# One link fewer before the flag, the spread of two integers as a 128-column product, a mask of GpSimd behind VectorE's, and one copy moved to VectorE

## The chip, the cores and the metric

The kernel runs on one core of a Trainium2 chip. The metric is the device time of one execution, in microseconds (us); lower is better. Engines are called TensorE (PE, with its weight loads as PEld), VectorE (DVE), ScalarE (ACT), GpSimd (POOL) and SyncE (SP, which here only issues transfers).

## What is computed

Attention followed by two feed-forward blocks, all in float32:

```python
scores = q @ k^T / sqrt(64)                   # 2 batches, 8 heads, 768 rows, head size 64
rel = i - j
keep = (j < n_global) | ((rel >= 0) & (rel < n_local))
dist = where(j < n_global and not local, n_local, |rel|)
scores = where(keep, scores - 2**-(h + 1) * dist, -1e9)     # h = 0..7, one slope per head
x = softmax(scores) @ v                       # reshaped to 1536 x 512
x = silu(x @ w_in1) @ w_out1                  # 512 -> 2048 -> 512
y = (h * clip(h + 3, 0, 6) / 6) @ w_out2, with h = x @ w_in2
```

n_global is 8 and n_local is 96, but they are int64 inputs that the kernel reads when it runs.

## The kernel before, in words

**Attention.** The 16 heads are 8 pairs; each pair has 6 tiles of 128 query rows. A unit u is one query tile of one pair of heads (48 units). Since only a band and a few global columns survive the mask, a unit computes 128 x 256 scores per head (128 x 128 in the first tile of a pair). This "banded" path holds if n_global is at most 32 and n_local is from 1 to 97; otherwise a "general" path runs. The choice is made on the device: VectorE computes a flag from the two integers, and every engine waits for it (`flag_ok`), loads it into a register and branches (`either`, L229 to L236).

**The start.** SyncE fetches the integers (L242). VectorE turns them into float32 (L531), writes three derived numbers in the same one-partition row (L532 to L534, each raising `row_ok`), and computes the flag in a chain of three dependent operations (L535, L536, L537), each waiting for the one before. TensorE multiplies idle tiles of ones meanwhile (L1058, four before and two behind), and between them the spread product (L1062): ones times a 128 x 5 tile `rows` whose first partition holds the five numbers, which puts them on all partitions. VectorE copies them from PSUM to `nums` (L544).

**The masks.** m_base holds, for each of 384 columns, minus eight times the distance or a very large negative number. VectorE makes its last 128 columns, OWN (L562, L564, L567, and L568 on 32 columns, which raises `own_ok`), and multiplies them by the slope of head 0 (L571). GpSimd makes the first 256, BAND (L427 on 32 columns, L430 on 256, and L433 on 32, which raises `band_ok`), with a clipped distance from ScalarE (L912). Then it multiplies them by the slope of head 1 (L436, `bias_band1`), and waits for own_ok before it makes the biases of the further heads (L330). VectorE multiplies BAND by the slope of head 0 (L575) after band_ok. ScalarE multiplies OWN by the slope of head 1 (L915) after own_ok.

**The flow of a unit.** TensorE's scores (L1088 for units 0 and 1, L1076 for two units at a time); VectorE's negation (L623), which adds the bias and takes the maximum, per head; ScalarE's exponential (L842), per head; TensorE's transposes of the probabilities (L1100) into one of two PSUM banks; a copy of these into probsT by ScalarE (L853) or VectorE (L636); TensorE's product with v (L1124). GpSimd prepares and spreads the inverse sums (L316, L324), TensorE turns them (L1109), ScalarE copies them (L858), and VectorE scales the outputs (L641). Transposes of unit u wait for the copy of unit u-2, and values wait for the copies of their own units. The helper `copied(u)` (L225) gives the semaphore and value of unit u's copy. VectorE copies the odd units from 3 on, ScalarE the even ones and unit 1.

**What sets the order.** Every engine's instructions are written out by hand, in `banded()` of each engine, and run strictly in that order; semaphores hold them back. The negation of unit u may start when the exponentials of unit u-3 are done, and scores of units 2r and 2r+1 when the negations of units 2r-2 and 2r-1 are.

**Feed-forward.** 32 steps, each of seven products of quarter matrices (L1152) and the product with w_out (L1234, L1243), on float32 split into a high and a low part. TensorE runs them back to back; VectorE, ScalarE and GpSimd split weights and apply the activation. The outputs are collected in y_out, which nothing uses before the second block, apart from the ones of the idle products (in y_out[:, 0, 0:128]).

Of the kernel before, what the change touches and what calls it, by code (L numbers as in the profile page):

```python
# [9 lines left out]
ALU = mybir.AluOpType  # L10
ACT = mybir.ActivationFunctionType

P = 128
# [11 lines left out]
GLOB = 32  # L25
KS = P + GLOB
KW = NT * KS - GLOB
MAXLOC = 97
MASKED = -1.0e9
NEVER = -1.0e30  # L30
# [41 lines left out]
def build(nc, qT, kT, v, w_in1, w_out1, w_in2, w_out2, counts, out):  # L72
    outer = ExitStack()
    with outer:
        def sb(name, shape, dt=F32, ctx=outer):
            return ctx.enter_context(nc.sbuf_tensor(name, shape, dt))
# [14 lines left out]
        wo_raw = sb("wo_raw", [P, 2, 2 * DM])  # L91
        ident = sb("ident", [P, P])
        words = sb("words", [1, 4], I32)
        rows = sb("rows", [P, 9])
        cnt = rows[0:1, :]
        nums = sb("nums", [P, 5])
        flag = sb("flag", [1, 1], I32)
        slope = sb("slope", [P, 2 * NH])
# [45 lines left out]
        g_hi = sb("g_hi", [P, 2, 2, 2 * TB], F32R)  # L144
        g_lo = sb("g_lo", [P, 2, 2, 2 * TB], F32R)
        y_out = sb("y_out", [P, NT, DM])

        ps = outer.enter_context(nc.psum_tensor("ps", [P, 8, 512], F32))

# [74 lines left out]

        def copied(u):  # L225

            return (pt_dve, u // 2) if u % 2 and u > 1 else (pt_act, u + 1 if u < 2 else u // 2 + 2)

        def either(eng, banded, general):  # L229

# [73 lines left out]
        def _(pool):  # L304
# [117 lines left out]
            def banded():  # L422

                key, far, glb = m_tmp[1], m_tmp[3], m_tmp[4]
                pool.wait_ge(nums_ok, 1)
                pool.wait_ge(iota_ok, MW_IOTAS)
                nc.gpsimd.tensor_scalar(glb[:, BAND_GLOB], key[:, BAND_GLOB], nums[:, 0:1], NEVER, ALU.is_ge,  # L427
                                        ALU.mult).then_inc(band_link, 1)
                pool.wait_ge(far_ok, 1)
                nc.gpsimd.tensor_tensor(m_base[:, BAND], rel8[:, BAND], far[:, BAND], ALU.subtract).then_inc(band_link, 1)  # L430

                pool.wait_ge(band_link, 2)
                nc.gpsimd.tensor_scalar(m_base[:, BAND_GLOB], glb[:, BAND_GLOB], nums[:, 3:4], 1.0, ALU.add,  # L433
                                        ALU.mult).then_inc(band_ok, 1)
                pool.wait_ge(band_ok, 1)
                nc.gpsimd.tensor_scalar(m_bias[:, 1, BAND], m_base[:, BAND], slope[:, 1:2], 1.0, ALU.mult,  # L436
                                        ALU.mult).then_inc(bias_band1, 1)
                pool.wait_ge(own_ok, 1)
                for r in range(NR):
                    if r < 3:  # L440
                        bias(2 * r + 2)
                        bias(2 * r + 3)
                    if r == 2:
                        spread(1)
                    elif r % 2 == 0 and r >= 4:
                        spread(r - 2)
                        spread(r - 1)
                    total(r)
                    if r == 1:
                        spread(0)  # L450
                    for kind, which, part in W_WORK.get(r, ()):
                        if kind == "s":
                            w_sum(which, part)
                        elif kind == "h":
                            w_high(which, part)
                        elif kind == "l":
                            w_low(which, part)
                        else:
                            wo_low(which)
                    for kind, which, half in X_WORK.get(r, ()):  # L460
                        if kind == "s":
                            x_sum(0, which, half)
                        elif kind == "h":
                            x_high(which)
                        else:
                            x_low(which)
                spread(NR - 2)
                spread(NR - 1)
                for n in (2, 3):
                    for half in range(2):  # L470
                        x_sum(0, n, half)
# [34 lines left out]
        def _(dve):  # L506
            links = [0]

            def link(ins):

                links[0] += 1
                ins.then_inc(chain, 1)
                dve.wait_ge(chain, links[0])

            nc.vector.memset(y_out[:, 0, 0:P], 1.0).then_inc(idle_ok, 1)
            nc.vector.memset(rows[:, 4:9], 0.0).then_inc(chain, 1)
            links[0] += 1
            for h in range(2 * NH):  # L520
                nc.vector.memset(slope[:, h:h + 1], 2.0 ** (-8.0 * (h % NH + 1) / NH)).then_inc(chain, 1)
# [7 lines left out]
            lowu = words[:, :].bitcast(U32).rearrange("p (n w) -> p n w", w=2)  # L529
            highi = words[:, :].rearrange("p (n w) -> p n w", w=2)  # L530
            link(nc.vector.scalar_tensor_tensor(cnt[:, 4:6], highi[:, :, 1], 4294967296.0, lowu[:, :, 0], ALU.mult, ALU.add))  # L531
            nc.vector.tensor_scalar(cnt[:, 6:7], cnt[:, 5:6], 0.0, None, ALU.max).then_inc(row_ok, 1)  # L532
            nc.vector.tensor_scalar(cnt[:, 7:8], cnt[:, 5:6], -8.0, 0.0, ALU.mult, ALU.min).then_inc(row_ok, 1)
            nc.vector.tensor_scalar(cnt[:, 8:9], cnt[:, 5:6], -0.5, -BEYOND, ALU.add, ALU.mult).then_inc(row_ok, 1)  # L534
            link(nc.vector.tensor_scalar(cnt[:, 0:1], cnt[:, 5:6], 1.0, None, ALU.is_ge))  # L535
            link(nc.vector.scalar_tensor_tensor(cnt[:, 0:1], cnt[:, 5:6], float(MAXLOC), cnt[:, 0:1], ALU.is_le, ALU.mult))  # L536
            nc.vector.scalar_tensor_tensor(flag[:, :], cnt[:, 4:5], float(GLOB), cnt[:, 0:1], ALU.is_le,  # L537
                                           ALU.mult).then_inc(flag_ok, 1)
            common = links[0]
            ng, nl = nums[:, 0:1], nums[:, 2:3]  # L540

            def numbers():
                dve.wait_ge(rows_ok, 1)
                nc.vector.tensor_copy(nums[:, :], ps[:, 1, 0:5]).then_inc(nums_ok, 1)  # L544
                dve.wait_ge(nums_ok, 1)

            def masks(link, rel, jj, loc, glb, keep, ngl, dist):
# [95 lines left out]
            def banded():  # L643
                numbers()
                base()

                def negations(r):
                    u = 2 * r
                    if u % NT == 0 and 0 < u < 4 * NT:
                        dve.wait_ge(bias_ok, 2 * (u // NT))  # L650
                    for k in (u, u + 1):
                        negated(k, 0)
                        negated(k, 1)

                negated(0, 0)
                dve.wait_ge(bias_own1, 1)
                negated(0, 1)
                band_bias()
                negated(1, 0)
                dve.wait_ge(bias_band1, 1)  # L660
                negated(1, 1)
                negations(1)
                inverse(0)
                negations(2)
                negations(3)
                inverse(1)
                copy_t(3)
                for m in range(2, NM):
                    negations(2 * m)
                    inverse(2 * m - 2)  # L670
                    if m == 2:
                        copy_t(4 * m - 3)
                    inverse(2 * m - 1)
                    negations(2 * m + 1)
                    if m > 2:
                        copy_t(4 * m - 3)
                    x_scaled(m - 2)
                    copy_t(4 * m - 1)
                inverse(NR - 2)
                inverse(NR - 1)  # L680
                x_low(0, T1)
                copy_t(NU - 3)
                x_scaled(NM - 2)
                x_low(0, B22)
                c_sum(0, 0, 1, p1_c, P2)
                copy_t(NU - 1)
                x_low(0, T3)
                x_low(0, T4)
                c_sum(0, 1, 0, p5_c, P7)
                silu(0, 0)  # L690
                c_sum(0, 2, 1, u2_c, P3)
                for n in range(1, 4):
                    silu(0, n)
                x_scaled(NM - 1)
# [131 lines left out]
        def _(act):  # L826
# [19 lines left out]
            def copy_t(u):  # L846
                act.wait_ge(pt_done, u + 1)
                at_least(act, pv_done, u // 2 - 2)
                src, dst = pt_bank(u), probsT[:, u % 6, :, :]
                if u % NT == 0:  # L850
                    src = src.rearrange("p (h a) k -> p h a k", h=2)[:, :, 1, :]
                    dst = dst.rearrange("p (h a) k -> p h a k", h=2)[:, :, 1, :]
                nc.scalar.activation(dst, src, ACT.Copy).then_inc(pt_act, 1)  # L853
# [55 lines left out]
            def banded():  # L909
# [10 lines left out]
                copy_t(1)  # L920
                exps(3)
                exps(4)
                copy_t(2)
                exps(5)
                exps(6)
                exps(7)
# [124 lines left out]
        def _(pe):  # L1051
# [3 lines left out]

            def busy(n):
                for _ in range(n):
                    nc.tensor.matmul(ps[:, 0, 0:P], y_out[:, 0, 0:P], y_out[:, 0, 0:P], start=True, stop=True)  # L1058

            busy(4)  # L1060
            pe.wait_ge(row_ok, 3)
            nc.tensor.matmul(ps[:, 1, 0:5], y_out[:, 0, 0:P], rows[:, 4:9], start=True, stop=True).then_inc(rows_ok, 1)  # L1062
            busy(2)
            pe.wait_ge(ident_ok, 2)

# [268 lines left out]
```

## Time and profile before

| | us |
|---|---|
| median of 3 runs | 587.07 (586.82 to 587.07) |
| the profiled execution's own time | 586.97 |
| its span, first to last instruction | 585.2 |
| TensorE busy in the span | 580.0 (99%) |
| VectorE busy | 361.9 (62%) |
| ScalarE busy | 335.5 (57%) |
| GpSimd busy | 266.7 (46%) |

The span is what the trace shows; the execution's own time has a little more around it. Busy time says how much of the span an engine had an instruction under way. It does not say what the others waited for: that is read from the chain of waits (followed back from the last instruction) and, where several engines work in turns, from the timeline. A fp32 product of TensorE appears as two records. The ends of TensorE's records are modelled, and its records overlap, as do those of VectorE and ScalarE by some hundredths where nothing is waited for.

### The profile page before, as it was taken

What the parts mean: (1) busy time and instruction counts of PE and PEld (TensorE: products, weight loads), DVE (VectorE), ACT (ScalarE), POOL (GpSimd) and SP (SyncE); (2) the same over time, 40 slices, a digit from 0 to 9 for tenths busy, and PEclk for the clock granted to TensorE, in tenths of its full rate; (3) what the DMA queues carried; (4) which work ended last, traced back from release to release, by engine and by line L of the source; (5) the groups of instructions that cost most, each with busy time, mean ns of one, the idle gap of its engine ahead of it and who ended that gap; (6) DMA issues with size and microseconds to landing.
All of it is one profiled execution on the core that took longest, in us unless ns stands there. A gap on an engine that the chain in (4) does not pass through costs nothing.

```text
span 585.2 us, 9670 instructions
## 1 busy us (share of the span) xinstructions
PE 580.0 (99%) x3476; PEld 522.5 (89%) x3476; DVE 361.9 (62%) x669; ACT 335.5 (57%) x652; POOL 266.7 (46%) x282
## 2 busy tenths in 40 slices
PE   9999999999999999999999999999999999999998
PEld 6788899999999999999999989999988988889996
DVE  7777887657545775586556685475448765555331
ACT  7998976554444774444447575445546754455441
POOL 6678774678333044394333343593330443331110
DMA  6665500422222122212221222222211262211002
GB/s 238 256 237 191 204 7 2 144 72 73 73 73 72 36 73 73 73 43 101 73 72 37 73 72 73 74 72 73 71 46 30 70 216 72 71 37 38 1 0 108
DMA packets 14883, 50.05 MB, mean 86 GB/s; under 512 B 1650, under 2 KB 2162, under 8 KB 14834
## 3 DMA queue, kind: packets, MB, share of 16 engines
q1 hardware_dynamic: 14402, 48.63, 24.5%
q10 hardware_dynamic: 432, 0.79, 0.4%
q8 instruction: 28, 0.46, 0.3%
q14 instruction: 21, 0.17, 0.1%
HBM read 46.27 MB, written 3.15 MB: 84 GB/s over the span
## 4 chain that ended last, share of the span: by engine, by line
PE 97%; DVE 1%; ACT 1%; issue 0%; DMA 0%; DVEq 0%
PE ps L1152 40%; PE ps L1243 23%; PE ps L1234 15%; PE ps L1235 8%; PE ps L1100 3%; PE ps L1124 3%; PE ps L1076 3%; PE ps L1109 1%; ACT probs L842 1%; DVE negs L623 0%; DMA words<-in_counts 0%; ACT probsT L853 0%; DVEq L232 0%; DVE m_base L568 0%; DVE x_raw L641 0%
## 5 line engine op out<-in xcount | busy, mean ns | idle before, releaser
L404 POOL TENSOR_TENSOR wo_lo<-wo_raw,wo_hi 128x1024 fp32r<-128x1024 f32 x32 | 77.3, 2415 | 260.1 <-ACT wo_hi L907 257.0
L1152 PE MATMUL ps<-x_hi,wi_hi 128*128 128x384 f32 x448 | 150.8, 337 | 0.1
L1152 PE MATMUL ps<-x_hi,wi_lo 128*128 128x384 f32 x448 | 150.0, 335 | 0.0
L1152 PE MATMUL ps<-x_lo,wi_hi 128*128 128x384 f32 x448 | 150.0, 335 | 0.0
L599 DVE TENSOR_TENSOR c_sb<-ps,p_c 128x384 f32<-128x384 f32 x64 | 35.6, 557 | 161.7 <-PE ps L1152 161.5
L887 ACT ACTIVATE p_c<-ps 128x384 f32<-128x384 f32 x64 | 31.5, 492 | 127.4 <-PE ps L1152 127.1
L1152 PEld LDWEIGHTS ps<-x_hi,wi_hi 128*128 128x128 f32 x448 | 84.1, 188 | 3.4 <-ACT u_c L887 0.9
L1152 PEld LDWEIGHTS ps<-x_hi,wi_lo 128*128 128x128 f32 x448 | 84.1, 188 | 0.7
L1152 PEld LDWEIGHTS ps<-x_lo,wi_hi 128*128 128x128 f32 x448 | 84.1, 188 | 0.0
L1243 PE MATMUL ps<-wo_hi,g_lo 128*128 128x512 f32 (+1 forms) x194 | 76.3, 393 | 0.0
L1243 PE MATMUL ps<-wo_lo,g_hi 128*128 128x512 f32 (+1 forms) x194 | 76.3, 393 | 0.0
L1243 PE MATMUL ps<-wo_hi,g_hi 128*128 128x512 f32 (+1 forms) x194 | 76.2, 393 | 0.0
L996 ACT ACTIVATE g_hi<-g_f 128x768 fp32r<-128x768 f32 x64 | 50.6, 838 | 42.3 <-DVE g_f L609 24.8
L581 DVE TENSOR_TENSOR wi_lo<-wi_raw,wi_hi 128x896 fp32r<-128x896 f32 x60 | 66.8, 1152 | 0.0
L865 ACT ACTIVATE wi_hi<-wi_raw 128x896 fp32r<-128x896 f32 x60 | 53.6, 937 | 0.0
L1234 PE MATMUL ps<-g_hi,wo_hi 128*128 128x512 f32 x128 | 50.0, 391 | 0.0
L1234 PE MATMUL ps<-g_lo,wo_hi 128*128 128x512 f32 x128 | 50.0, 391 | 0.0
L1234 PE MATMUL ps<-g_hi,wo_lo 128*128 128x512 f32 x128 | 50.0, 390 | 0.0
L842 ACT ACTIVATE probs<-negs,negmax 128x256 f32<-128x256 f32 (+1 forms) x96 | 45.8, 481 | 3.8 <-DVE negmax L623 3.7
L1243 PEld LDWEIGHTS ps<-wo_hi,g_lo 128*128 128x128 f32 x194 | 36.4, 188 | 8.6
L1243 PEld LDWEIGHTS ps<-wo_hi,g_hi 128*128 128x128 f32 x194 | 36.4, 188 | 8.0
L1243 PEld LDWEIGHTS ps<-wo_lo,g_hi 128*128 128x128 f32 x194 | 36.5, 188 | 8.0
(113 smaller groups left out, 1064.3 us busy)
## 6 DMA issues: line engine op xcount, KB each, us to landing
wi_raw<-in_w_in SPq DMA_DIRECT2D x32, 512.0 KB, 3.4
wo_raw<-in_w_out SPq DMA_DIRECT2D x32, 512.0 KB, 3.4
v_raw<-in_v SPq DMA_DIRECT2D x8, 704.0 KB, 4.0
k_raw<-in_kT SPq DMA_DIRECT2D x7, 464.0 KB, 5.1
out_y<-y_out SPq DMA_DIRECT2D x11, 256.0 KB, 4.1
q_raw<-in_qT SPq DMA_DIRECT2D x6, 384.0 KB, 6.0
q_raw<-in_qT ACTq DMA_DIRECT2D x1, 384.0 KB, 4.6
k_raw<-in_kT SPq DMA_DIRECT2D x1, 320.0 KB, 3.7
```

Of the source, the lines that this page charges most:

```text
L404: nc.gpsimd.tensor_tensor(wo_lo[:, s % 2, :], wo_raw[:, s % 2, :], wo_hi[:, s % 2, :], ALU.subtract).then_inc(wo_lo_ok, 1)
L581: nc.vector.tensor_tensor(wi_lo[:, s % 2, at], wi_raw[:, s % 2, QC + 7 * P * part:QC + 7 * P * part + 7 * P], wi_hi[:, s % 2, at], ALU.sub ...
L599: nc.vector.tensor_tensor(c_sb[:, i, :], p_bank(bank), add[:, :], ALU.add).then_inc(c_ok, 1)
L842: nc.scalar.activation(probs[:, u % DEEP, h, a:256], negs[:, u % 3, h, a:256], ACT.Exp, bias=negmax[:, u % DEEP, h:h + 1], scale=-1.0, acc ...
L865: nc.scalar.activation(wi_hi[:, s % 2, at], wi_raw[:, s % 2, QC + 7 * P * part:QC + 7 * P * part + 7 * P], ACT.Copy).then_inc(wi_hi_ok, 1)
L887: nc.scalar.activation(dst[:, :], p_bank(bank), ACT.Copy).then_inc(kept, 1)
L996: nc.scalar.activation(g_hi[:, s % 2, f, :], g_f[:, f, :, :].rearrange("p a t -> p (a t)"), ACT.Copy, scale=1.0 if s < NSTEP // 2 else 1.0 ...
L1076: mm = nc.tensor.matmul(s_bank(u, h)[:, 0:width], q_raw[it % 2][D * h:D * h + D, P * t:P * t + P], k_raw[it % 2][D * h:D * h + D, first:fi ...
L1152: mm = nc.tensor.matmul(p_bank(bank), w[:, s % 2, at], x[:, b, k, :], start=fresh and k == 0 and i == 0, stop=k == 1 and i == 2, skip_grou ...
L1234: nc.tensor.matmul(y_bank(i), wo[:, s % 2, w], g[:, s % 2, c, 0:512], start=first, stop=last)
L1235: mm = nc.tensor.matmul(y_bank(4 + i // 2)[:, 256 * (i % 2):256 * (i % 2) + 256], wo[:, s % 2, w], g[:, s % 2, c, 512:S], start=first and ...
L1243: mm = nc.tensor.matmul(y_bank(t)[:, cols], g[:, s % 2, c, P * t:P * t + P], wo[:, s % 2, DM * c + cols.start:DM * c + cols.stop], start=s ...
```

## The change

VectorE computes two tests side by side, 98 - n_local and (n_global > 32) times 1e30, and makes the flag from both and n_local in one operation: flag = ((98 - n_local) x n_local > second test). Both tests are issued ahead of the three row operations. The row tile is 128 columns wide and lies in y_out, like the ones; the spread product is 128 columns wide and has three idle products ahead of it instead of four. GpSimd waits for own_ok ahead of L430 instead of ahead of the further biases. The copy of unit 2 goes from ScalarE, where it stood behind the exponentials of unit 4, to VectorE, where it stands between the negations of units 5 and 6.

```diff
-        rows = sb("rows", [P, 9])
-        cnt = rows[0:1, :]
+        tests = sb("tests", [1, 2])
...
+        ones, rows = y_out[:, 0, 0:P], y_out[:, 1, 0:P]
+        cnt = y_out[0:1, 1, 0:P]
...
         def copied(u):
-            return (pt_dve, u // 2) if u % 2 and u > 1 else (pt_act, u + 1 if u < 2 else u // 2 + 2)
+            if u in (0, 1):
+                return pt_act, u + 1
+            if u == 2:
+                return pt_dve, 1
+            return (pt_dve, u // 2 + 1) if u % 2 else (pt_act, u // 2 + 1)
...
                 pool.wait_ge(far_ok, 1)
+                pool.wait_ge(own_ok, 1)
                 nc.gpsimd.tensor_tensor(m_base[:, BAND], rel8[:, BAND], far[:, BAND], ALU.subtract).then_inc(band_link, 1)
...
-                pool.wait_ge(own_ok, 1)
                 for r in range(NR):
...
-            nc.vector.memset(y_out[:, 0, 0:P], 1.0).then_inc(idle_ok, 1)
-            nc.vector.memset(rows[:, 4:9], 0.0).then_inc(chain, 1)
+            nc.vector.memset(ones, 1.0).then_inc(idle_ok, 1)
+            nc.vector.memset(rows, 0.0).then_inc(chain, 1)
...
+            nc.vector.tensor_scalar(tests[:, 0:1], cnt[:, 5:6], -1.0, MAXLOC + 1.0, ALU.mult, ALU.add).then_inc(chain, 1)
+            nc.vector.tensor_scalar(tests[:, 1:2], cnt[:, 4:5], float(GLOB), -NEVER, ALU.is_gt, ALU.mult).then_inc(chain, 1)
+            links[0] += 2
             nc.vector.tensor_scalar(cnt[:, 6:7], cnt[:, 5:6], 0.0, None, ALU.max).then_inc(row_ok, 1)
             nc.vector.tensor_scalar(cnt[:, 7:8], cnt[:, 5:6], -8.0, 0.0, ALU.mult, ALU.min).then_inc(row_ok, 1)
             nc.vector.tensor_scalar(cnt[:, 8:9], cnt[:, 5:6], -0.5, -BEYOND, ALU.add, ALU.mult).then_inc(row_ok, 1)
-            link(nc.vector.tensor_scalar(cnt[:, 0:1], cnt[:, 5:6], 1.0, None, ALU.is_ge))
-            link(nc.vector.scalar_tensor_tensor(cnt[:, 0:1], cnt[:, 5:6], float(MAXLOC), cnt[:, 0:1], ALU.is_le, ALU.mult))
-            nc.vector.scalar_tensor_tensor(flag[:, :], cnt[:, 4:5], float(GLOB), cnt[:, 0:1], ALU.is_le,
-                                           ALU.mult).then_inc(flag_ok, 1)
+            dve.wait_ge(chain, links[0])
+            nc.vector.scalar_tensor_tensor(flag[:, :], tests[:, 0:1], cnt[:, 5:6], tests[:, 1:2], ALU.mult,
+                                           ALU.is_gt).then_inc(flag_ok, 1)
...
-                nc.vector.tensor_copy(nums[:, :], ps[:, 1, 0:5]).then_inc(nums_ok, 1)
+                nc.vector.tensor_copy(nums[:, :], ps[:, 1, 4:9]).then_inc(nums_ok, 1)
...
                 negations(2)
+                copy_t(2)
                 negations(3)
...
                 exps(4)
-                copy_t(2)
                 exps(5)
...
-                    nc.tensor.matmul(ps[:, 0, 0:P], y_out[:, 0, 0:P], y_out[:, 0, 0:P], start=True, stop=True)
-            busy(4)
+                    nc.tensor.matmul(ps[:, 0, 0:P], ones, ones, start=True, stop=True)
+            busy(3)
             pe.wait_ge(row_ok, 3)
-            nc.tensor.matmul(ps[:, 1, 0:5], y_out[:, 0, 0:P], rows[:, 4:9], start=True, stop=True).then_inc(rows_ok, 1)
+            nc.tensor.matmul(ps[:, 1, 0:P], ones, rows, start=True, stop=True).then_inc(rows_ok, 1)
             busy(2)
```

## Rows read from the trace of the kernel before

**Rows 1.** The page: TensorE's busy time, and the chain that ended last, by engine.

```profile
PE 580.0 (99%) x3476; PEld 522.5 (89%) x3476; DVE 361.9 (62%) x669; ACT 335.5 (57%) x652; POOL 266.7 (46%) x282
PE 97%; DVE 1%; ACT 1%; issue 0%; DMA 0%; DVEq 0%
```

**Rows 2.** Windows of TensorE: stretch, its length, busy, PEclk, DMA share, GB/s.

```profile
20.00:100.00 80.00, 79.71 (x768) 1.00 0.39 139
```

**Rows 3.** Timeline, 2 to 4 us: start, length, engine, line, operation, shapes, idle before.

```profile
2.27 0.14 DVE L532 TENSOR_SCALAR rows<-rows 1x1 f32<-1x1 f32 x1
2.34 0.13 DVE L533 TENSOR_SCALAR rows<-rows 1x1 f32<-1x1 f32 x1
...
2.81 0.15 DVE L537 SCALAR_TENSOR_TENSOR flag<-rows 1x1 int32<-1x1 f32 x1
...
2.99 0.43 PE L1062 MATMUL ps<-rows,y_out 128*128 128x5 f32 x2
...
3.27 1.20 PE L1058 MATMUL ps<-y_out 128*128 128x128 f32 x4
...
3.98 0.16 DVE L544 COPY nums<-ps 128x5 f32<-128x5 f32 x1 [1.03 <-PE ps L1062]
```

**Rows 4.** The chain of waits at 3 us: start, length, what.

```profile
3.00 0.54 DVEq L232
```

**Rows 5.** Timeline, 4.3 to 6.8 us, VectorE and GpSimd.

```profile
4.38 0.23 DVE L564 TENSOR_SCALAR x_t<-x_t,nums 128x32 f32<-128x32 f32 x1
...
4.89 0.73 POOL L430 TENSOR_TENSOR m_base<-x_t 128x256 f32<-128x256 f32 x1
4.98 0.68 DVE L568 SCALAR_TENSOR_TENSOR m_base<-x_t,nums,m_base 128x32 f32<-128x32 f32 x1
...
5.70 0.29 DVE L571 TENSOR_SCALAR m_bias<-m_base,slope 128x128 f32<-128x128 f32 x1
5.72 0.34 POOL L433 TENSOR_SCALAR m_base<-x_t,nums 128x32 f32<-128x32 f32 x1
...
6.16 0.48 POOL L436 TENSOR_SCALAR m_bias<-m_base,slope 128x256 f32<-128x256 f32 x1
...
6.44 0.35 DVE L575 TENSOR_SCALAR m_bias<-m_base,slope 128x256 f32<-128x256 f32 x1
```

**Rows 6.** Timeline, 10 to 19 us: the rows on which the handover turns.

```profile
10.41 0.66 PE L1100 MATMUL ps<-ident,probs 128*128 128x128 f32 x4
...
11.40 0.29 DVE L623 CUSTOM_DVE_ANT_0 negs<-ps,m_bias 128x128 f32<-128x128 f32 x1 [0.85 <-ACT probs L842]
...
12.12 0.58 ACT L853 ACTIVATE probsT<-ps 128x512 f32<-128x512 f32 x1
12.24 0.42 DVE L623 CUSTOM_DVE_ANT_0 negs<-ps,m_bias 128x256 f32<-128x256 f32 x1 [0.33 <-ACT probs L842]
...
12.59 0.50 ACT L842 ACTIVATE probs<-negs,negmax 128x256 f32<-128x256 f32 x1
...
13.03 0.66 DVE L636 COPY probsT<-ps 128x512 f32<-128x512 f32 x1
...
15.33 0.58 ACT L858 ACTIVATE inverses<-ps 128x512 f32<-128x512 f32 x1
...
16.01 1.75 PE L1124 MATMUL ps<-probsT,v_raw 128*64 128x128 f32 x28 [0.34 <-issue]
...
17.41 0.42 DVE L623 CUSTOM_DVE_ANT_0 negs<-ps,m_bias 128x256 f32<-128x256 f32 x1 [0.26 <-ACT probs L842]
...
18.10 0.69 DVE L641 TENSOR_TENSOR x_raw<-ps,inverses 128x512 f32<-128x512 f32 x1
...
18.93 0.63 PE L1109 MATMUL ps<-ident,rinv 128*128 128x128 f32 x4 [0.37 <-DVE x_raw L641]
```

**Rows 7.** Score products by line and shape, 5.84 to 7.5 us, then 7.85 to 9 us.

```profile
L1076 PE MATMUL ps<-k_raw,q_raw 64*128 64x256 f32 x8 | 1.7, 589 | 0.0
...
L1076 PE MATMUL ps<-k_raw,q_raw 64*128 64x256 f32 x8 | 1.1, 402 | 0.0
```

## What I expected before the changed kernel ran

> **What bounds the kernel now.** I read the page first. TensorE is busy for 580.0 us of a span of 585.2 us, and the chain that ended last is 97% TensorE [rows 1]. The reader is to see that nearly the whole time is one engine's work, which this change leaves alone: it takes one idle product out of the first 4 us and makes a 5-column product 128 columns wide. Next I cut the span into stretches. From 20 to 100 us TensorE is busy for 79.71 of 80.00 us [rows 2], so of its 5.2 idle us only 0.29 lie in those 80 us, and behind that come the same products back to back. So a microsecond can only be won before about 19 us, where TensorE still waits for others; what is won there moves all that follows, one for one, because afterwards the matmul queue is full and only slides.
>
> Then I followed the chain of waits and the timeline through those 19 us. They have three parts. Up to 3.98 us: the integers arrive, a chain of one-element VectorE operations makes the flag at 2.81, VectorE reads the flag and branches (a 0.54 us piece from 3.00), and copies the spread numbers at 3.98 [rows 3, 4]. From 3.98 to 6.79: the masks, up to the bias of unit 1's first head, L575 [rows 5]. Then ScalarE exponentiates and copies without a pause, and hands over to TensorE between 13 and 19 us [rows 6].
>
> **The change part by part.**
>
> *Integers to flag.* Now: L531, three row operations from 2.27, then two dependent links, then the flag at 2.81 [rows 3]. Independent one-element operations start 0.07 apart (2.27, 2.34). Afterwards five of them stand between L531 and the flag: 2.27 + 5 x 0.065 = 2.60. The flag's own wait is for the second test, started 2.34 and lasting 0.13, so over at 2.47: no stall. The flag comes 0.21 earlier, and with it the branch of VectorE: 3.98 - 0.21 = 3.77 for the copy of the numbers, if the spread is there. The wider memset of the row tile falls before the integers have arrived, where VectorE has nothing else to do, so it costs nothing; without that cover it would be at most 0.29, what L571 takes for 128 columns [rows 5].
>
> *The spread.* The last row operation ends 0.13 later than now, since two tests stand before it: at 2.66 instead of 2.53. Today the spread product starts at 2.99, right behind idle products; with three ahead of it instead of four it waits for its row rather than for the array. Today it starts 0.46 after its row is ready; with the same distance it starts near 3.12 (2.85 if that distance was the array's doing). It is now as wide as an idle product, two of which (four records) take 1.20, so it takes about 0.6 and ends near 3.75, against 2.99 + 0.43 = 3.42 now [rows 3]. That is just where the branch puts the copy. I take the copy at 3.82, a gain of 0.16; bounds 0.21 (spread early enough) and a loss of 0.1 (the wide product 0.3 later than I think, half its own length). TensorE's first scores gain nothing: three wide idle products and the wide spread fill what four and a narrow one filled. They have slack anyway: VectorE first reads them behind L571, which ends at 5.99.
>
> *GpSimd behind VectorE.* This is the largest local saving. L568 works on 32 columns like L564, which took 0.23, but took 0.68. It started at 4.98 while GpSimd's L430 ran (4.89 + 0.73 = 5.62) and ended at 5.66, just behind it [rows 5]. So it was held up for about 0.45. The Trainium skill (SBUF — State Buffer, "Who interferes with whom") says that a VectorE instruction with two inputs in SBUF and a GpSimd instruction that reads SBUF exclude one another for a whole instruction; the trace agrees with it in this pair. With L430 behind own_ok, L568 starts at 4.82 and ends at 5.06 instead of 5.66: VectorE wins 0.60. But GpSimd loses: L430 started at 4.89 and now starts at 5.08 at the earliest. Queued behind it are L433 and L436 (and all its later biases, which have slack: they are for units 6 and later). L430 ends at 5.81, L433 starts 0.1 later and takes up to 0.34: band_ok at 6.25. VectorE's L575 waits for band_ok. Today it starts at 6.44, held up by VectorE's own queue (band_ok came at 6.06). Afterwards VectorE's queue would reach it at about 5.85, so band_ok is what is late next: L575 starts at 6.28, 0.16 earlier. Bounds: L433 has no competing VectorE operation beside it any more, and may take 0.1 less (a gain of 0.3); or L430 is held up by L571, which becomes ready at the same moment and lasts 0.29 [rows 5] (a loss of 0.13). I take a gain of 0.15. Of VectorE's 0.6, most is waited away.
>
> *Unit 2's copy.* ScalarE's copy at 12.12 is 0.58 long and moves its successor by 0.47 (12.12 to 12.59) [rows 6]. It goes from the busiest engine of this stretch. VectorE takes it over ahead of negation 6: the transposes of unit 2 end at 10.41 + 0.66 = 11.07, and a copy of this size takes 0.66 on VectorE. Today VectorE idles there for 0.85 until 11.40, then does unit 6 and idles again for 0.33 until 12.24 [rows 6]. So unit 6's two negations take 12.24 - 0.33 - 11.40 = 0.51. With the copy from 11.10 to 11.76 they are done at 12.27, when unit 7 may just start. VectorE pays 0.03, at worst 0.1; without those two gaps it would pay 0.6. ScalarE then starts unit 5 at 12.12 and ends unit 7 at 14.86 instead of 15.33. Its copy of the inverses ends at 15.44 instead of 15.91, so TensorE's values, which sat idle for 0.34 before 16.01, start when the transposes leave the array, about 0.45 earlier. Unit 8 follows on ScalarE and is done 0.4 earlier, so VectorE's negation at 17.41, ahead of which it sat idle for 0.26 on ScalarE, moves by 0.26 to 0.3 (today negations start a little before their forerunner's record ends), and so does the scaling of x at 18.10. TensorE's turn of the inverses, idle for 0.37 for that scaling, moves from 18.93 to 18.63 [rows 6]. This is where the gain is banked: 0.3. Bounds: 0.1 (VectorE, which also carries copies 3 and 5, becomes the limit) and 0.45.
>
> *Transfers and queues.* No load is reordered. SyncE's later loads hang on score and value products and are issued some tenths earlier; none is in the chain after the integers.
>
> **Sum.** 0.15 + 0.3 = 0.45 us. The profiled execution took 586.97 (span 585.2, so 1.8 lies around it) and should take about 586.5. It stands 0.1 below the median of the runs shown, 587.07, so the median should become 586.6, a change of 0.08%. About 0.2% (1.2 us) is what a measurement of this kernel can tell from no change: my forecast is well inside it.
>
> **The rivals.**
>
> *A collision moved, not removed.* own_ok now releases L571 on VectorE and L430 on GpSimd together. If one holds up the other by its 0.29 or 0.73, band_ok comes at about 6.55 and L575 is no earlier than today; the prologue gives nothing and only the copy's 0.3 is left: 586.75. For it: L568's 0.68 shows that the two engines do block one another. Against: L575 and L571 read one tile from SBUF, not two, and L575 took 0.35 beside GpSimd's L436. The skill's same section says that a fp32 tensor_scalar can use both ports and then collides too; by it this rival holds.
>
> *Everything is absorbed.* The negations and copies of VectorE, or a transfer, limit TensorE again before 19 us; the result is 587.0. For it: VectorE carries unit 3's copy at 13.03 and unit 5's after it, and the latter stands behind TensorE's transposes, not behind ScalarE. Against: the idle times at 16.01, 17.41 and 18.93 all lie downstream of ScalarE [rows 6].
>
> *All in full:* 0.3 + 0.45 = 0.75, giving 586.3.
>
> *Slower: TensorE's clock rises later.* The granted clock is printed as 1.00 everywhere, but the score products took 589 ns in the mean from 5.84 to 7.5 us and 402 ns from 7.85 us on [rows 7]; the first are at 1.2 GHz, the second at 2.4. The array had been given work with hardly a break since the first idle product. The change opens a gap of some 0.5 us before the spread product. If the rise falls behind scores 2 and unit 1's transposes, eight score records take 1.7 instead of 1.1 us [rows 7], and four transposes 1.2 (as four idle records do [rows 3]) instead of 0.66 [rows 6]: 0.6 + 0.5 = 1.1 where ScalarE's copy of unit 1 waits for just those. Net +0.65: 587.7. If it comes only after scores 5, two more groups of scores at 0.6 are added and it is near 589. It decides once the rise slips beyond 9 us. Against: the idle work is nearly the same, only its order differs.
>
> *The change does not do what it says* is not open: every part is plain in the order of instructions.
>
> **How the numbers follow.** Forecast (586.4 to 586.75) 0.50; collision 0.19; absorbed 0.13; all in full 0.08; late clock 0.07 near 587.7 and 0.03 near 589. The range takes in the bounds of both terms and the first late-clock case: 586.1 to 587.8. Slower by over 0.2% needs 588.2, the second late-clock case and a little besides: 0.04. Faster by over 0.2% needs 1.2 us, more than both terms at their upper bounds: 0.03. The rest, 0.93, is within 0.2%.
>
> **What would show it.** Right: flag at about 2.60, numbers at about 3.8, L568 at some 0.25 us, L575 near 6.3 with VectorE idle before it for GpSimd, ScalarE's unit 5 directly behind unit 4, values near 15.4 and the turn of the inverses near 18.5 (both terms together). Wrong: L571 or L430 stretched by 0.3 or more; score products at 589 ns after 8 us; idle time on VectorE or TensorE between 13 and 19 us that the trace of before does not have; or a shift at 20 us that is not found again at 580 us.

## The result and the profile after

The changed kernel takes 583.00 us (median of 6 runs, 582.98 to 583.01) against 586.90 us for the kernel before (median of 6 runs, 586.82 to 587.07). The ratio is 0.9933 (95% interval 0.9920 to 0.9946): 3.9 us or 0.67% faster. I had forecast 0.45 us, counted from 587.07, the median of the three runs that I had then. The mechanism that I wrote down is in the trace, and its sum is worth about what I said, though one of its two terms was smaller and the other larger; 3.4 us more come from something that my sum did not contain.

First the places that I had named. The timeline of the changed kernel, up to 7 us:

```profile
2.33 0.13 DVE L542 TENSOR_SCALAR tests<-y_out 1x1 f32<-1x1 f32 x1
...
2.57 0.20 DVE L548 SCALAR_TENSOR_TENSOR flag<-tests,y_out 1x1 int32<-1x1 f32 x1
...
2.70 0.80 PE L1073 MATMUL ps<-y_out 128*128 128x128 f32 x2
...
3.79 0.16 DVE L555 COPY nums<-ps 128x5 f32<-128x5 f32 x1 [1.02 <-PE ps L1073]
...
4.79 0.25 DVE L579 SCALAR_TENSOR_TENSOR m_base<-x_t,nums,m_base 128x32 f32<-128x32 f32 x1
...
5.19 0.76 POOL L439 TENSOR_TENSOR m_base<-x_t 128x256 f32<-128x256 f32 x1 [0.25 <-DVE m_base L579]
...
6.05 0.29 POOL L442 TENSOR_SCALAR m_base<-x_t,nums 128x32 f32<-128x32 f32 x1
...
6.38 0.35 DVE L586 TENSOR_SCALAR m_bias<-m_base,slope 128x256 f32<-128x256 f32 x1 [0.47 <-POOL m_base L442]
```

Flag at 2.57 (forecast 2.60; before 2.81), numbers at 3.79 (forecast 3.82). L579, the old L568, takes 0.25 instead of 0.68 [rows 5]. And VectorE now sits idle for 0.47 for GpSimd before L586, which starts at 6.38 against 6.44: of some 0.6 us freed on VectorE, 0.06 are left.

The handover to TensorE, 10 to 19 us, answering to [rows 6]:

```profile
10.80 0.69 DVE L647 COPY probsT<-ps 128x512 f32<-128x512 f32 x1 [0.35 <-PE ps L1111]
...
12.06 0.42 DVE L634 CUSTOM_DVE_ANT_0 negs<-ps,m_bias 128x256 f32<-128x256 f32 x1 [0.15 <-ACT probs L854]
...
14.67 0.59 ACT L870 ACTIVATE inverses<-ps 128x512 f32<-128x512 f32 x1
...
15.42 1.75 PE L1135 MATMUL ps<-probsT,v_raw 128*64 128x128 f32 x28
...
17.57 0.69 DVE L652 TENSOR_TENSOR x_raw<-ps,inverses 128x512 f32<-128x512 f32 x1
...
18.41 0.63 PE L1120 MATMUL ps<-ident,rinv 128*128 128x128 f32 x4 [0.43 <-DVE x_raw L652]
```

The values start without idle time at 15.42 (16.01 before), and the turn of the inverses at 18.41 (18.93 before). So at 19 us the changed kernel is 0.52 us ahead. But its span is 581.3 us against 585.2, 3.9 us shorter. Behind 20 us no idle time has gone: TensorE is busy for 79.72 of the 80 us (79.71 before [rows 2]), and over the whole span it is idle for 5.2 us in both kernels (581.3 less 576.1 us busy; 585.2 less 580.0).

```profile
20.00:100.00 80.00, 79.72 (x767) 1.00 0.39 139
```

So the products themselves must have become shorter. The page of each kernel has a row for every kind of product. In the second block, g is the stationary operand (128 columns) and w_out the moving one (512 columns). Changed kernel first, then before:

```profile
L1254 PE MATMUL ps<-wo_hi,g_lo 128*128 128x512 f32 (+1 forms) x194 | 75.3, 388 | 0.0
L1254 PE MATMUL ps<-wo_lo,g_hi 128*128 128x512 f32 (+1 forms) x194 | 75.3, 388 | 0.0
L1254 PE MATMUL ps<-wo_hi,g_hi 128*128 128x512 f32 (+1 forms) x194 | 75.0, 387 | 0.0
```

```profile
L1243 PE MATMUL ps<-wo_hi,g_lo 128*128 128x512 f32 (+1 forms) x194 | 76.3, 393 | 0.0
L1243 PE MATMUL ps<-wo_lo,g_hi 128*128 128x512 f32 (+1 forms) x194 | 76.3, 393 | 0.0
L1243 PE MATMUL ps<-wo_hi,g_hi 128*128 128x512 f32 (+1 forms) x194 | 76.2, 393 | 0.0
```

The same 582 products add up to 75.3 + 75.3 + 75.0 = 225.6 us against 76.3 + 76.3 + 76.2 = 228.8 us, 3.2 us apart. These sums are not the time that the block takes, since each record runs on beside its successor's. From the start of each product to the start of the next, these products take 131.1 us against 134.3, again 3.2 us apart. The products of g and w_out in the first block take 133.1 us against 133.3. With the 0.52 us of the start, that is the whole 3.9 us. The diff touches no instruction there. One by one, in the same stretch of a step (476 us; changed kernel, then before):

```profile
475.87 0.39 PE L1254 MATMUL ps<-wo_lo,g_hi 128*128 128x512 f32 x1
476.10 0.39 PE L1254 MATMUL ps<-wo_hi,g_lo 128*128 128x512 f32 x1
476.33 0.39 PE L1254 MATMUL ps<-wo_hi,g_hi 128*128 128x512 f32 x1
476.55 0.39 PE L1254 MATMUL ps<-wo_lo,g_hi 128*128 128x512 f32 x1
476.78 0.39 PE L1254 MATMUL ps<-wo_hi,g_lo 128*128 128x512 f32 x1
```

```profile
475.94 0.40 PE L1243 MATMUL ps<-wo_hi,g_lo 128*128 128x512 f32 x1
476.17 0.40 PE L1243 MATMUL ps<-wo_hi,g_hi 128*128 128x512 f32 x1
476.40 0.40 PE L1243 MATMUL ps<-wo_lo,g_hi 128*128 128x512 f32 x1
476.63 0.40 PE L1243 MATMUL ps<-wo_hi,g_lo 128*128 128x512 f32 x1
476.87 0.40 PE L1243 MATMUL ps<-wo_hi,g_hi 128*128 128x512 f32 x1
```

The reader should look at the starts, since the ends are modelled: four products further is 0.91 us in the changed kernel and 0.93 us before. Over all pairs of neighbours in this block the mean distance of starts is 225.7 ns against 231.0 ns.

**What else had changed.** The row tile of 9 columns is gone and a tile of 2 columns has come. In the compiled program the tiles lie one behind the other, each rounded up to 32 bytes per partition: 36 bytes took 64, 8 bytes take 32. So every tile allocated behind it moved down by 32 bytes, g_hi from 176032 to 176000 and g_lo from 188320 to 188288, while x, w_in's parts and w_out's parts (wo_hi at 112768) stayed. The *address theory* is that this is worth the 3.4 us. Its rival: the start leaves the engines or the transfers in another phase, which lasts.

### The profile page after: what moved, and what is told of

Same layout as the page of the kernel before. It is cut to its first block, busy times and chain, and to the rows that moved or that the text cites. A ratio compares the mean times of both kernels' runs of the same rounds, so it can differ in the third digit from the quotient of the medians.

```text
span 581.3 us, 9667 instructions
## 1 busy us (share of the span) xinstructions
PE 576.1 (99%) x3474; PEld 521.1 (90%) x3474; DVE 361.5 (62%) x670; ACT 335.0 (58%) x651; POOL 266.9 (46%) x282
## 4 chain that ended last, share of the span: by engine, by line
PE 97%; DVE 1%; ACT 1%; issue 0%; DMA 0%; POOL 0%; DVEq 0%; POOLq 0%
PE ps L1163 40%; PE ps L1254 23%; PE ps L1245 15%; PE ps L1246 8%; PE ps L1111 3%; PE ps L1135 3%; PE ps L1087 3%; PE ps L1120 1%; ACT probs L854 1%; DVE negs L634 0%; DMA words<-in_counts 0%; DVEq L239 0%; POOL m_base L439 0%; ACT probsT L865 0%; DVE x_raw L652 0%
## 5 line engine op out<-in xcount | busy, mean ns | idle before, releaser
L1254 PE MATMUL ps<-wo_hi,g_lo 128*128 128x512 f32 (+1 forms) x194 | 75.3, 388 | 0.0
L1254 PE MATMUL ps<-wo_lo,g_hi 128*128 128x512 f32 (+1 forms) x194 | 75.3, 388 | 0.0
L1254 PE MATMUL ps<-wo_hi,g_hi 128*128 128x512 f32 (+1 forms) x194 | 75.0, 387 | 0.0
```

Of the source, the lines that this page charges most:

```text
L1254: mm = nc.tensor.matmul(y_bank(t)[:, cols], g[:, s % 2, c, P * t:P * t + P], wo[:, s % 2, DM * c + cols.start:DM * c + cols.stop], start=s ...
```

## The experiments

Every run was compared with the kernel before on the same chip, whose median was 586.84 to 586.89 us. "Pad" is an unused tile, such as

```diff
         warm = sb("warm", [P, 1])
+        sb("pad", [P, 8])
```

which moves the tiles behind it by 32 bytes (`[P, 32]`: 128 bytes) and changes no instruction. "Up" means to higher addresses. Distances are those between g_hi and wo_hi; g_lo and wo_lo have the same remainders by 256 bytes, unless it is said.

### First round: is it the places, and whose?

*The kernel before, 32 bytes up* (the pad above).

> The kernel before with one unused tile of 32 bytes per partition behind warm: no instruction differs, but q_raw0, g_hi, g_lo, y_out and all else behind it lie 32 bytes further (g_hi at 176064 instead of 176032, a multiple of 64). Address theory (the 3.4 us that the changed kernel wins behind 19 us come from the 32 bytes by which its layout moved): 583.5 (586.9 less 3.4), and the product L1243 starts every 226 ns instead of 231. Rival (they come from the start: another phase between engines, transfers or the clock that lasts): no change, 586.9.

589.27 us (ratio 1.0041, 1.0027 to 1.0055): neither 583.5 nor 586.9. A pad with no instruction in it costs 2.4 us, so places matter; but g_hi at a multiple of 64 is not what makes the products fast. The first form of the address theory fell. The products of the second block start every 231.0 ns, just as before; 2.2 of the 2.4 us lie in the first block's products of g and w_out (135.5 us from start to start in all, 133.3 before). One row of this run, and its like in the changed kernel (391 ns; 390 in the kernel before):

```profile
L1235 PE MATMUL ps<-g_hi,wo_lo 128*128 128x512 f32 x128 | 50.9, 398 | 0.0
```

```profile
L1245 PE MATMUL ps<-g_hi,wo_lo 128*128 128x512 f32 x128 | 50.0, 391 | 0.0
```

*The changed kernel, 32 bytes up* (the same pad), so that its tiles lie where they lay before.

> The changed kernel with the same 32-byte pad, so that everything behind warm lies where it lay before. What is left is the change of the program itself. Address theory: 586.4 (586.9 less the 0.5 seen at 18.4 us). Rival: stays at 583.0.

586.45 us (11 runs, 586.37 to 586.56; before 586.86; ratio 0.9993, 0.9984 to 1.0002). The 3.4 us are gone, with the whole change of the program still in. Its page shows the products of before to the digit:

```profile
L1255 PE MATMUL ps<-wo_hi,g_lo 128*128 128x512 f32 (+1 forms) x194 | 76.3, 393 | 0.0
L1255 PE MATMUL ps<-wo_lo,g_hi 128*128 128x512 f32 (+1 forms) x194 | 76.3, 393 | 0.0
L1255 PE MATMUL ps<-wo_hi,g_hi 128*128 128x512 f32 (+1 forms) x194 | 76.2, 393 | 0.0
```

*Only g up* (the pad directly ahead of g_hi).

> The changed kernel with the pad directly ahead of g_hi: only g_hi, g_lo and y_out go back to their old places, the attention's tiles and g_f stay. Address theory with g as the operand that matters: 586.2 to 586.4, L1254 every 231 ns. If it were the attention's tiles or g_f, c_sb and gate: 583.0 to 583.3. Rival (start): 583.0.

586.41 us (0.9992, 0.9983 to 1.0002), with the same three rows. The tiles that matter are g_hi and g_lo (y_out moved too, but is no operand there); the attention's tiles, g_f, c_sb and gate are not.

*Only g_lo up* (the pad between g_hi and g_lo).

> The pad between g_hi and g_lo: only g_lo and y_out move by 32 bytes. In the second block g is the stationary operand, g_hi in two of three products, g_lo in one. If a product pays for its own stationary operand's address, only one in three pays: 583.0 + 3.1/3 = 584.0. If the whole row of products pays as soon as one operand is off: 586. If it was y_out's place: 586 too, and g_hi's products slow as the rest.

587.37 us (1.0013, 1.0003 to 1.0022), worse than with both up, and so worse than either branch of my expectation. The excess over both up does not lie in the second block (230.8 ns from start to start in the mean, 231.0 with both up) but in the first, where a product of 512 columns and its companion of 256 take 350.8 ns together, against 347.2. Its rows contradict the idea that a product pays for its own operand:

```profile
L1255 PE MATMUL ps<-wo_lo,g_hi 128*128 128x512 f32 (+1 forms) x194 | 76.9, 396 | 0.0
L1255 PE MATMUL ps<-wo_hi,g_hi 128*128 128x512 f32 (+1 forms) x194 | 76.1, 392 | 0.0
L1255 PE MATMUL ps<-wo_hi,g_lo 128*128 128x512 f32 (+1 forms) x194 | 75.1, 387 | 0.0
```

The product with the moved g_lo is the fastest (387), and the one issued directly ahead of it, wo_lo with g_hi, the slowest (396). While a product runs, the weights of the next are loaded (in the changed kernel, beside the product at 476.10 us, from 476.10 on for 0.19 us). So this looks as if a product paid for the place of its successor's stationary operand against its own moving one. That is a reading of one run, not a test of it, and it leaves a row open: wo_hi with g_hi took 392 instead of 387, though neither its operands nor its successor's had moved.

### Second round: relative or absolute, and with what period?

*The kernel before, 32 bytes down.*

```diff
-        three = sb("three", [P, 1])
-        warm = sb("warm", [P, 1])
+        three_warm = sb("three_warm", [P, 2])
+        three, warm = three_warm[:, 0:1], three_warm[:, 1:2]
```

> The kernel before with three and warm as two columns of one tile: no instruction differs, the tiles behind them move 32 bytes down, just as in the changed kernel (g_hi at 176000). The run with 32 bytes up was slower (589.3), so it is not a 64-byte boundary as such. Theory (g's place relative to wo_hi and wo_lo, which did not move: the distance g_hi - wo_hi is 63232 bytes, a multiple of 128 and 256): 583.4, that is 586.9 less 3.4. Rival (the changed program is needed for it as well): 586.9.

583.47 us (0.9942, 0.9928 to 0.9956), as expected. Not one instruction differs from the kernel before, and 3.4 of the 3.9 us are there:

```profile
L1243 PE MATMUL ps<-wo_hi,g_lo 128*128 128x512 f32 (+1 forms) x194 | 75.3, 388 | 0.0
L1243 PE MATMUL ps<-wo_lo,g_hi 128*128 128x512 f32 (+1 forms) x194 | 75.3, 388 | 0.0
L1243 PE MATMUL ps<-wo_hi,g_hi 128*128 128x512 f32 (+1 forms) x194 | 75.0, 387 | 0.0
```

*Every tile 32 bytes up* (the pad ahead of x_raw).

> The changed kernel with the pad ahead of x_raw, the first tile: every tile moves by 32 bytes, so distances stay (63232) and only absolute addresses change. If the distance between g and wo decides: 583.0. If the absolute address of g decides (g_hi at 176032, as before): 586.4.

582.99 us (0.9933, 0.9918 to 0.9948). g_hi is again at 176032, where it is slow in the kernel before, and is fast. So for this shift the absolute addresses do not matter; distances do.

*128 bytes, 96 bytes and 256 bytes behind warm.*

> The changed kernel with 128 bytes behind warm: the distance g_hi - wo_hi is a multiple of 128 but not of 256. If the pattern repeats every 128 bytes: 583.0. If every 256 or more: above 585.

587.43 us (1.0016, 1.0006 to 1.0025).

> The changed kernel with 96 bytes behind warm, g 32 bytes short of a multiple of 128. If only a distance that is a multiple of 128 is fast and any other slow: 586 to 589, like 32 (586.4) and 64 (589.3 with the program of before, so 588.9 with this one). If it is the bytes beyond a multiple that cost in order 32, 64, 96: above 589.

588.53 us (1.0027, 1.0016 to 1.0038).

> The changed kernel with 256 bytes behind warm: the distance g_hi - wo_hi is again a multiple of 256 (248 times). The shifts so far: 0 gave 583.0, 32 gave 586.45, 96 gave 588.5, 128 gave 587.4. If the pattern repeats every 256 bytes: 583.0. If only that one distance happened to be good: above 585.

583.08 us (0.9936, 0.9921 to 0.9951), with the rows of the changed kernel. All this together, as times of the changed program (for 64 bytes the program of before, 589.27, less the 0.4 by which the two differ at 32 bytes; this 588.9 is an estimate, and its two distances are those of the program of before). In the first block a product of 512 moving columns and its companion of 256 are taken together:

| distance g to wo, remainder by 256 bytes | us | second block, mean start distance, ns | first block, 512 and 256 columns together, ns |
|---|---|---|---|
| 0 (the changed kernel; also 256 bytes) | 583.0 (583.1) | 225.7 | 346.7 |
| 32 (the places of before) | 586.45 | 231.0 | 347.2 |
| 64 | about 588.9 | 231.0 | 352.8 |
| 96 | 588.5 | 232.0 | 350.2 |
| 128 | 587.4 | 230.1 | 350.8 |

A remainder of 0 is clearly best of the five; 160, 192 and 224 were not tried. From 0 to 32 bytes it is nearly all the second block that pays; beyond 32 bytes the first block pays as well. In these runs g moved against x and w_in too, so the last column does not tell which of the distances it goes by.

### Third round: the parts of the program, one at a time

All three at the layout of before. Each differs from 586.85 by a few tenths, and each ratio's interval contains 1; what I read is medians of 11 runs each, and traces.

*The copy alone* (with `copied` as in the change).

```diff
...
                 negations(2)
+                copy_t(2)
                 negations(3)
...
                 exps(4)
-                copy_t(2)
                 exps(5)
```

> The kernel before with unit 2's copy moved to VectorE and nothing else; g_hi stays at 176032. By my prediction's own step 0.3 us: 586.6. If the copy is worth less than that because VectorE or TensorE limits again: 586.8 or more. The whole program change is worth 0.43 at this layout (586.88 less 586.45).

586.48 us (586.43 to 586.78; ratio 0.9993, 0.9984 to 1.0002): 0.37 us less, against 0.3 expected. The trace shows why: the values have lost their idle time, and the turn of the inverses starts at 18.48 (18.93 in [rows 6]).

```profile
15.49 1.75 PE L1128 MATMUL ps<-probsT,v_raw 128*64 128x128 f32 x28
17.17 0.88 PE L1104 MATMUL ps<-ident,probs 128*128 128x128 f32 x6
18.48 0.63 PE L1113 MATMUL ps<-ident,rinv 128*128 128x128 f32 x4 [0.43 <-DVE x_raw L645]
```

*The order of the masks alone.*

```diff
                 pool.wait_ge(far_ok, 1)
+                pool.wait_ge(own_ok, 1)
...
-                pool.wait_ge(own_ok, 1)
                 for r in range(NR):
```

> The kernel before with GpSimd's wait for own_ok ahead of L430 and nothing else. In the changed kernel's trace band_ok became the late one: L586 started at 6.38 with the numbers copied 0.19 earlier than before. With the numbers at 3.98 again it would start at 6.57, 0.13 later than the 6.44 of before: 587.0. If VectorE's freed 0.4 us were worth something by itself: below 586.8.

587.00 us (586.92 to 587.67; ratio 1.0003, 0.9994 to 1.0012): 0.15 more. In this execution the integers came some 0.2 late, so distances count: L568 is short again, and VectorE has 0.47 of idle time for GpSimd ahead of L575.

```profile
5.22 0.25 DVE L568 SCALAR_TENSOR_TENSOR m_base<-x_t,nums,m_base 128x32 f32<-128x32 f32 x1
...
6.81 0.35 DVE L575 TENSOR_SCALAR m_bias<-m_base,slope 128x256 f32<-128x256 f32 x1 [0.47 <-POOL m_base L434]
```

From L568's start to L575's are 1.59 us; before they were 6.44 - 4.98 = 1.46 [rows 5]. By itself this edit loses 0.13 by this measure. The measure is rough: in the traces of the next run and of the one ahead, which have the old order, the distance is 1.56 and 1.39, because the integers came at 2.16 and 2.17 there, while GpSimd's first mask operation started at 4.40 and 4.39 as before, and its later ones set the time. The other way to read it is 6.81 less the 0.21 by which the integers were late (2.30 against 2.09), which is 6.60, 0.16 behind 6.44; the medians say 0.15.

*The shorter chain alone*: the two tests and the flag as in the change, the tests in unused columns of the row tile, with the narrow spread and four idle products.

```diff
         cnt = rows[0:1, :]
+        tests = rows[0:1, 0:2]
...
```

> The kernel before with the two tests in unused columns of the row tile and the shorter chain, narrow spread and four idle products as before. The changed kernel's trace shows GpSimd's L434 at 4.41 although the numbers came at 3.79, so GpSimd is held by its own branch and L430 would still end at 5.62. L568 then ends behind it as before, and the earlier flag is worth nothing: 586.9. If the flag moves all that follows: 586.7.

586.90 us (586.74 to 587.30; ratio 1.0000, 0.9991 to 1.0010). VectorE's and GpSimd's rows show where the earlier flag goes:

```profile
2.65 0.20 DVE L540 SCALAR_TENSOR_TENSOR flag<-rows 1x1 int32<-1x1 f32 x1
...
4.87 0.78 DVE L571 SCALAR_TENSOR_TENSOR m_base<-x_t,nums,m_base 128x32 f32<-128x32 f32 x1
...
6.43 0.35 DVE L578 TENSOR_SCALAR m_bias<-m_base,slope 128x256 f32<-128x256 f32 x1
```

```profile
4.88 0.72 POOL L431 TENSOR_TENSOR m_base<-x_t 128x256 f32<-128x256 f32 x1
```

The mask operation starts 0.11 earlier (4.87 against 4.98) and takes 0.10 longer (0.78 against 0.68). It ends at 5.65, behind GpSimd's 4.88 + 0.72 = 5.60, as it did before. The chain's gain is eaten by the collision; taking the collision away loses some 0.15 on GpSimd's side; both together give the 0.06 seen at L586 of the changed kernel (no run has these two without the copy). With that, the parts add up: -0.37 for the copy, -0.06 for the other two, -0.43, against 586.86 - 586.45 = 0.41 for the whole program at one layout, and 583.47 - 583.00 = 0.47 at the other. The wide spread and its three idle products were not tried alone; they are inside this sum.

### Fourth round: which pair?

*wo and g up, against x and w_in* (the pad ahead of wo_hi).

> The changed kernel with 32 bytes ahead of wo_hi: wo and g move together, x and wi stay. If the two operands of one product must lie a multiple of 256 bytes apart: 583.0. If g must agree with x or wi as well: about 586.4.

*All but x up* (the pad ahead of wi_hi).

> The changed kernel with 32 bytes ahead of wi_hi: x stays, wi, wo and g move together. The pair rule says that L1254 stays at 226 ns and L1163 (1344 products of wi with x) pays instead: at 2 to 6 ns each 585.7 to 591. If only products with w_out are sensitive: 583.0.

584.84 us (0.9965, 0.9951 to 0.9979) and 584.86 us (0.9966, 0.9953 to 0.9978): between the two expectations of each. The products of the second block stay fast, even a little faster than in the changed kernel (224.7 ns from start to start in both), so for them the distance of g and wo is enough. L1164, the products of x and w_in, pays nothing for 32 bytes between its operands in the run with all but x up (174.8 ns from start to start in the mean, 174.9 in the changed kernel), so the rule does not hold for every product. What pays are the wide products of the first block, where w_out is stationary and g moves:

```profile
L1246 PE MATMUL ps<-g_lo,wo_hi 128*128 128x512 f32 x128 | 51.6, 403 | 0.0
L1246 PE MATMUL ps<-g_hi,wo_hi 128*128 128x512 f32 x128 | 50.9, 398 | 0.0
L1246 PE MATMUL ps<-g_hi,wo_lo 128*128 128x512 f32 x128 | 50.6, 395 | 0.0
```

That is the page of the run with wo and g up; in the changed kernel all three took 391 ns. In the run with all tiles moved g and wo had the very same addresses, and these products took 391. So the first block's products depend on where x (or something else ahead of w_in) lies, though they do not read it, and the distance of g and wo is not enough for them. The products of x directly precede them, but if they left something behind, one would expect it to fade, and the trace of the run with wo and g up shows no fading: in a stretch of such products the sixth of 512 columns starts its companion 241.1 ns later, and the thirty-sixth 240.5 ns (230 for both in the changed kernel). Why distances matter at all, and how x comes in, stays open.

## Why the prediction was wrong

**The step that failed** is the sentence "nearly the whole time is one engine's work, which this change leaves alone". The change issues no other instruction there, but it moves g, one of the two operands of TensorE's products with w_out, by 32 bytes. That a microsecond could only be won before about 19 us fell with it. With that term missing, the sum was -0.45 instead of -3.9, and the range ended at 586.1. The program's own part is -0.41 to -0.47, measured at two layouts; the layout's is 586.89 - 583.47 = 3.42. Of that, 3.2 lie in the second block and 0.2 in the first. The prediction had named the sign of it: "a shift at 20 us that is not found again at 580 us"; the shift was 0.52 us near 19 us and 3.9 at the end. No row of the kernel before prices a shifted operand, but the diff shows the cause openly: a tile taken out in the middle of the allocations. I read its memset's cost and not its place. "Forecast, collision, absorbed, in full, late clock" were all about the first 19 us, so the cases shared one blind spot, and the 0.93 for a result within 0.2% was as sure as it was because of it.

**The sum of the two terms**: close, in part by luck. 0.45 were forecast and 0.41 to 0.47 measured, but the masks gave 0.06 instead of 0.15, and the copy 0.37 instead of 0.3.

**Integers to flag**: right. 2.57 against 2.60.

**The spread**: right in its effect, but not by my reason. It started at 2.70, not at 3.12 or 2.85, 0.06 behind its row, and ended at 3.50, so it had 0.29 of slack to the copy. The 0.46 of before was the array's doing, and the spread does not set the copy's time.

**GpSimd behind VectorE**: the sign and the mechanism right, the size less: 0.06 at L586 instead of 0.16. L439 started 0.15 behind the end of L579, which raises own_ok (0.02 assumed), and took 0.76 (0.73 assumed); L442 followed it by 0.1 as assumed, and took 0.29 of the 0.34 allowed. L582 was not stretched (0.29), and L439 by at most 0.03, so the rival of a moved collision did not come true in this pair. At L586 it shows a little: GpSimd's L445, which started 0.06 behind it, took 0.64 against 0.48 for its counterpart L436 [rows 5], with no effect on the chain.

```profile
6.44 0.64 POOL L445 TENSOR_SCALAR m_bias<-m_base,slope 128x256 f32<-128x256 f32 x1
```

The Trainium skill (SBUF — State Buffer, "Who interferes with whom") has it that a tensor_scalar of VectorE can enter a mode that uses both ports, if its operands meet the conditions, and that GpSimd is then fully blocked where VectorE was first. This row agrees as to who waits, by 0.16 us; L582's neighbour does not show it: L439 ran beside L582 for 0.18 us and took 0.03 longer than L430.

**Unit 2's copy**: right. VectorE's copy from 10.80 to 11.49 fitted into its idle time, unit 7 started when ScalarE let it, and values started at 15.42 ("near 15.4"). Alone it gave 0.37 (0.3 forecast).

**The late clock**: did not happen, rather the reverse. The same score products took 477 ns in the mean against 589 [rows 7], so the array was at 2.4 GHz for more of them. (A product's start follows the one before by 0.43 us at first and by 0.21 later.)

```profile
L1087 PE MATMUL ps<-k_raw,q_raw 64*128 64x256 f32 x8 | 1.4, 477 | 0.0
```

In the run with the copy alone, whose start is that of the kernel before, they took 451. The other traces say the same: in the run of the changed kernel with 32 bytes behind warm a score product of this shape that started at 6.72 us still took 631 ns, and in the run with 96 bytes one that started at 4.60 took 378, though both run the same instructions. So this varies from execution to execution, and I can't credit the wide spread with it.

## What to carry to other kernels

When a diff adds, removes or resizes an on-chip tile, compare the addresses of all operands of the bounding engine before and after, and treat a shift as a change of its own: pad it back and measure. Here 32 bytes were worth seven to eight times as much as the edited instructions, and the sign can be either. When two engines collide, a shorter chain into the collision gives nothing, and removing the collision alone can lose; read what the second engine is late for before adding up savings.

## What the runs showed that I had not expected

- In the second block (512 moving columns, operands in the kernel's F32R type) the pace of the products depends on the distance between their operands: 225.7 ns from start to start if g and w_out lie a multiple of 256 bytes apart, 230 to 232 ns at remainders of 32, 64, 96 and 128. Distances count, not addresses: with all tiles moved by 32 bytes the time stayed at 582.99 us.
- In the first block the distance of g and w_out is not all: with the distance of g and w_out kept, but both 32 bytes further from x, the products of 512 columns took up to 403 ns instead of 391, and the kernel 584.84 instead of 582.99 us.
- With not one instruction changed, the places of its tiles moved the kernel before between 583.47 and 589.27 us, 1.0%.
- Moving one of two operands that alternate (g_lo without g_hi) was worse than moving both: 587.37 against 586.41 us. In the second block the slow product was then the one ahead of the moved operand's (396 ns), not its own (387 ns).
